# Second MoE of a fused attention and MoE kernel: the first unit's layer one is placed ahead of the other expert's folding, and fewer constant products stand among the first MoE's weight pieces

## The chip, the cores and the metric

The kernel runs on one core of a Trainium2 chip. It is one program: attention, a soft MoE over its output, and a top-1 MoE over that. The metric is the device time of one execution in microseconds (us), median of several runs; lower is better. TensorE (PE) does the matrix products, VectorE (DVE) and ScalarE (ACT) the elementwise work and the copies out of PSUM, GpSimd (POOL) some elementwise work and the indirect DMAs, SyncE (SP) issues the weight loads.

## The reference

```python
def _moe_ref(x, phi, w1, w2):            # first MoE, 8 experts, 4 slots each
    logits = x @ phi                     # x is the attention output, 3072 x 512
    d = softmax of logits over the tokens
    slot_input = (d.T @ x).reshape(E, S_per_e, D)
    for e in range(E):
        slot_out[e] = np.maximum(slot_input[e] @ w1[e], 0.0) @ w2[e]
    c = softmax of logits over the slots
    return c @ slot_out.reshape(n_slots, D)

def _moe2_ref(x, w_gate, w1, w2):        # second MoE, 8 experts, top 1
    logits = x @ w_gate
    expert_idx = np.argmax(logits, axis=1)
    gate_w = softmax(logits)[token, expert_idx]
    for e in range(E):
        mask = expert_idx == e           # experts without tokens are skipped
        out[mask] = gate_w[mask, None] * (np.maximum(x[mask] @ w1[e], 0.0) @ w2[e])
    return out
```
(shortened: the softmaxes are written in words.) w1 is 512 x 1024 and w2 is 1024 x 512 for each expert; each is 2 MB.

## The kernel before

**The first MoE's end.** Its weights come as 16 pieces of 2 MB (pieces 0 to 15), in order, through a ring of ten slots. Pieces 0 to 3 and 8 to 11 are first-layer weights (products at line 910), 4 to 7 and 12 to 15 second-layer weights (line 938). SP issues a load once its slot is free; a piece's products wait for its slot in `here(i)`. Ahead of that wait, for the pieces from 10 on, `here` issues 14 products of two constant tiles (`busy(14)`, line 836), whose result nobody reads. A product of f32 tiles shows in the trace as two records, so 14 of them read as x28 and 8 products of a piece as x16. After the last piece come ACT's copy of the result, four small products (line 954) and DVE's copy into `STR`, the 32 slot outputs.

**The second MoE's input is never formed.** A token's input is c (32 weights) times the slot outputs, so an expert's first layer is folded: G = slot outputs @ w1 of the expert, 32 rows (held as high and low parts in 128 partitions), and a token tile's hidden values are c @ G. Routing (DVE, lines 1607 to 1685) finds the experts in use, sorts the tokens by expert and makes units of 256 tokens, two tiles each. With this input two experts are in use, and there are 13 units. The weight loads (`v1`, first layer; `v2`, second layer) start when the experts are known, in the order v1 of expert 0, v1 of expert 1, v2 of expert 0, v2 of expert 1.

What PE does in order, with the lines of the kernel before:

1. `sort` (line 1411), 24 products with 42 columns: the tokens' numbers in sorted order. POOL then gathers the unit's rows of c from DRAM (line 1364, two indirect DMAs of 128 rows a unit).
2. Folding of both experts: per expert 8 products (line 1461), ACT copies the two halves out (line 1511), 2 products add the parts (line 1467), ACT writes the high part (line 1514), DVE the low part (line 1708).
3. `turn(0)` (line 1419), which transposes the gathered rows; the sort's second half with the gates (line 1411, 84 columns); `hidden(0)` (line 1427), the first unit's layer one. It waits for ACT's copy of the turned rows (line 1520) and of G into `Gst` (`fetch`, line 1540).
4. For each unit: tile 0 of the second layer, 24 products (lines 1490 to 1492) in four groups of six; inside it `turn(u + 1)`; after it `hidden(u + 1)`; then tile 1, 24 products. A group of tile 0 waits for its quarter of the hidden values (ACT's relu, line 1528, then DVE's low part, line 1714) and, with a new expert, for its quarter of the weights in high and low part (`high_in_place` on ACT, line 1551; `rest_in_place` on DVE, line 1721).

ACT and DVE have their orders written out by hand as well. On ACT, after the folding: `turned_out(0)`, `fetch(0)`, then the high parts of expert 0's second layer between the four relus, `fetch(e1)`, the four high parts of expert 1, and only then the loop over units, which begins with `turned_out(1)`. On DVE: routing, gates (lines 1688 to 1698), low parts of the folding, then low parts of hidden values and weights in turn, the final gates (1731, 1732), four low parts of expert 1's weights, and the loop over units.

Of the kernel before, what the change touches and what calls it, by code (L numbers as in the profile page):

```python
# [15 lines left out]
F32 = mybir.dt.float32  # L16
# [7 lines left out]
P = 128  # L24
# [646 lines left out]
def soft_moe(nc, ctx, sb, psum, sem, block, attended, mem, xmem, X, ident, ones, Rsel, phi_sb, load_piece,  # L671
# [134 lines left out]
    def _(pe):  # L806
# [327 lines left out]
def top1_moe(nc, ctx, sb, psum, sem, block, sp_passed, ident, ones, Rsel, wg_sb, mem, STR, CT, counting,  # L1134
# [27 lines left out]
    hh, hl = [work[:, i * HC:(i + 1) * HC].rearrange("p (q t) -> p q t", q=4) for i in range(2)]  # L1162
# [41 lines left out]
    sf = sb(st, "sf", [P, 3, MAXT])  # L1204

# [3 lines left out]
    def first_weights(odd):  # L1209

        return w2h[:, 1, :].bitcast(F32) if odd else raw
# [29 lines left out]
    v1_loaded = [sem("v1_loaded_even"), sem("v1_loaded_odd")]  # L1241
# [16 lines left out]
    g_here = sem("g_here")  # L1258
    act_passed = sem("act_passed")
# [20 lines left out]
    def count(eng):  # L1280

        return eng.value_load(rt[0:1, 5, 0:1], min_val=1, max_val=NE)
# [23 lines left out]
    def pairs_of(used):  # L1306


        return (used + 1) >> 1

    def load_v1(sp, e, odd):

        sp.dma_start(first_weights(odd).rearrange("p (c f) -> p c f", c=DC),
                     v1_d[bass.ds(e, 1)].rearrange("a (c p) f -> p (a c) f", p=P)).then_inc(v1_loaded[odd], 16)

    @block.sync
    def _(sp):
        sp.wait_ge(experts_known, 1)
        for odd in range(2):
            load_v1(sp, entry(sp, odd, 0), odd)  # L1320
        for r in range(2):
            load_v2(sp, entry(sp, r, 0), w2l[:, r, :].bitcast(F32), v2_loaded[r])
        used = count(sp)
        with sp.If(used > 2):
            with sp.Fori(1, pairs_of(used)) as i:
                for odd in range(2):
                    e = entry(sp, i * 2 + odd, 0)

                    sp.wait_ge(gp_done, i * 4 + 2 * odd)
                    sp.sem_inc(sp_passed, 1)  # L1330
                    load_v1(sp, e, odd)
            with sp.Fori(2, used) as r:
                e = entry(sp, r, 0)

                sp.wait_ge(w2_low, r * W2CH)
                sp.sem_inc(sp_passed, 1)
                load_v2(sp, e, raw, v2_loaded[1])

    @block.gpsimd
    def _(pool):  # L1340
        pool.sem_inc(y_quarter, 4)
        pool.sem_inc(y_scaled, 2)
        pool.sem_inc(gp_done, 2)
        pool.sem_inc(g_low, 2)
# [56 lines left out]
    def _(pe):  # L1401
# [20 lines left out]
        def hidden(u):  # L1422

            pe.wait_ge(cgt_out, u + 1)
            pe.wait_ge(g_here, u + 1)
# [25 lines left out]


        used = count(pe)
        with pe.Fori(0, pairs_of(used)) as i:
            pe.wait_ge(g_low, i * 4 + 2)
            for odd in range(2):
                pe.wait_ge(v1_loaded[odd], (i + 1) * 16)
                for half in range(2):
                    for c in range(DC):
                        at = c * F + half * 512  # L1460
                        mm = pe.matmul(Gp[c * SLOTS:(c + 1) * SLOTS, 2 * odd + half, :], STR[:, c, 0, :],
                                       first_weights(odd)[:, at:at + 512], start=True, stop=True,
                                       tile_position=(0, c * SLOTS))
                    mm.then_inc(gp_done, 1)
                for half in range(2):
                    pe.wait_ge(gp_out, i * 4 + 2 * odd + half + 1)
                    pe.matmul(Gp[:, 2 * odd + half, :], Rsel[:].rearrange("p r s -> p (r s)"),
                              Gpart[:, 2 * odd + half, :], start=True, stop=True).then_inc(g_done, 1)
        turn(0)
        pe.wait_ge(gates_hot, 1)  # L1470
        sort(slice(1, 3), slice(MAXT, 3 * MAXT))
        pe.wait_ge(g_low, pairs_of(used) * 4 + 2)
        hidden(0)
        pe.wait_ge(rt_ready, 1)
        with pe.Fori(0, used) as rank:
            units, first = entry(pe, rank, 1), entry(pe, rank, 2)
            high, low = [w[:, bass.ds(rank & 1, 1), :].rearrange("p a f -> p (a f)") for w in (w2h, w2l)]
            with pe.Fori(0, units) as j:

                u = first + j  # L1480
                for i in range(2):
                    pe.wait_ge(y_scaled, u * 2 + (i + 1))
                    for fc in range(FC):
                        if i == 0 and fc % 2 == 0:
                            pe.wait_ge(hid_low, u * 4 + (fc // 2 + 1))
                            pe.wait_ge(w2_low, rank * W2CH + (fc * D // CW + 1))
                        cols = slice(fc * D, (fc + 1) * D)
                        tokens = slice(fc % 2 * 2 * P + i * P, fc % 2 * 2 * P + (i + 1) * P)
                        h, rest = hh[:, fc // 2, tokens], hl[:, fc // 2, tokens]
                        pe.matmul(Yq[i][:], h, high[:, cols], start=(fc == 0), stop=False)  # L1490
                        pe.matmul(Yq[i][:], h, low[:, cols], start=False, stop=False)  # L1491
                        mm = pe.matmul(Yq[i][:], rest, high[:, cols], start=False, stop=(fc == FC - 1))  # L1492
                        if i == 0 and fc == 1:
                            turn(u + 1)
                        if i == 1 and fc % 2:
                            mm.then_inc(y_quarter, 1)
                    if i == 0:
                        mm.then_inc(y_first, 1)
                        hidden(u + 1)

    @block.scalar
    def _(act):
# [4 lines left out]
        with act.Fori(0, pairs_of(used)) as i:  # L1507
            for odd in range(2):
                for half in range(2):
                    act.wait_ge(gp_done, i * 4 + 2 * odd + half + 3)  # L1510
                    nc.scalar.copy(Gpart[:, 2 * odd + half, :], Gp[:, 2 * odd + half, :]).then_inc(gp_out, 1)
                for half in range(2):
                    act.wait_ge(g_done, i * 4 + 2 * odd + half + 1)
                    nc.scalar.copy(Gall[:, bass.ds(rank_at(i * 2 + odd), 1), half * 512:(half + 1) * 512].rearrange(
                        "p a f -> p (a f)").bitcast(F32R), Gp[:, 2 * odd + half, :]).then_inc(g_high, 1)
# [27 lines left out]
        act.wait_ge(rt_ready, 1)  # L1543
        e1 = act.value_load(tr[0:1, 1:2], min_val=0, max_val=NE - 1)
        act.wait_ge(g_low, pairs_of(used) * 4 + 2)
        act.sem_inc(act_passed, 1)

# [5 lines left out]

        turned_out(0)
        fetch(0)
        high_in_place(0, 0)
        for q in range(4):
            relu(0, q)
            if q < 3:
                high_in_place(0, q + 1)  # L1560
        fetch(e1)
        for ch in range(W2CH):
            high_in_place(1, ch)
# [21 lines left out]
    def _(dve):  # L1585
# [100 lines left out]

        dve.wait_ge(r_exp, 1)
# [12 lines left out]
        used = count(dve)  # L1700
        with dve.Fori(0, pairs_of(used)) as i:
            for odd in range(2):
                for half in range(2):
                    dve.wait_ge(g_high, i * 4 + 2 * odd + half + 1)
                    dve.sem_inc(dve_passed, 1)
                    rest = Gall[HD:P, bass.ds(rank_at(i * 2 + odd), 1), half * 512:(half + 1) * 512].rearrange(
                        "p a f -> p (a f)")
                    v.tensor_tensor(rest.bitcast(F32R), Gp[HD:P, 2 * odd + half, :], rest, ALU.subtract
                                    ).then_inc(g_low, 1)

        def low(u, q):

            dve.wait_ge(hid_high, u * 4 + (q + 1))
            v.scalar_tensor_tensor(hl[:, q, :], Gp[:, q, :], 0.0, hh[:, q, :].bitcast(F32),  # L1714
                                   ALU.max, ALU.subtract).then_inc(hid_low, 1)

        def rest_in_place(r, ch):

            dve.wait_ge(w2_high, r * W2CH + ch + 1)
            w = w2l[:, r, chunk(ch)]  # L1720
            v.tensor_tensor(w, w.bitcast(F32), w2h[:, r, chunk(ch)].bitcast(F32), ALU.subtract).then_inc(w2_low, 1)  # L1721

        for q in range(4):
            if q == 0:
                low(0, 0)
            rest_in_place(0, q)
            if q < 3:
                low(0, q + 1)
# [83 lines left out]
```

## Time and profile before

| | us |
|---|---|
| median of 3 runs | 462.95 (462.3 to 464.25) |
| profiled execution | 462.75 |
| its span in the trace | 461.0 |
| PE busy | 441.8 (96%) |
| DVE busy | 240.2 (52%) |
| ACT busy | 213.7 (46%) |
| POOL busy | 203.4 (44%) |

The page's line of the granted TensorE clock reads, over 40 equal slices of 11.5 us, `9999999999999999999999897799999999999999` in tenths of full speed. The span begins with the first instruction and ends with the last; the device time holds 1.75 us more around it. A busy PE may be waiting in the sense that matters: products of constant tiles count as busy. In a row of the trace the columns are start, length, engine, line, operation, result and operands, and in brackets the idle time ahead of it and what ended it. Records of PE overlap, since its ends are modelled; the chain of waits counts each stretch once.

### The profile page before, as it was taken

To read this page: it belongs to the slowest core of one execution; us is meant where nothing else is said; L and a number is where in the kernel's file an instruction comes from. 1 tells how busy PE (TensorE), PEld (TensorE's weight loads), DVE (VectorE), ACT (ScalarE), POOL (GpSimd) and SP (SyncE) were. 2 spreads that over 40 slices of the span, in tenths; PEclk is the share of its full clock that TensorE was granted. 3 is DMA by queue.
4 is the path that set the end of the run, shared out by engine and by line. 5 is a ranking of instruction groups with operands and counts; after the bars stand their busy time and mean duration, and the time that the engine had idled before them with its cause. 6 is when DMAs were issued, how large, how long until landed. Compare 5 with 4: busy or idle time off the path is not lost.

```text
span 461.0 us, 9685 instructions
## 1 busy us (share of the span) xinstructions
PE 441.8 (96%) x3152; PEld 370.7 (80%) x3153; DVE 240.2 (52%) x789; ACT 213.7 (46%) x419; POOL 203.4 (44%) x170
## 2 busy tenths in 40 slices
PE   8799999999999997999999989799999999999994
PEld 8689999999999995543567883688888888888883
DVE  6467677777677764665000386764333333333344
ACT  2578878788878763311010003853333232332243
POOL 3999888888888600020001001234333333333322
PEclk9999999999999999999999897799999999999999
DMA  8699898977676206999995059411111111111211
GB/s 233 261 411 370 338 386 305 381 267 253 213 254 217 66 2 204 383 401 408 390 384 162 1 202 383 169 36 57 57 57 57 57 57 45 46 57 54 54 49 13
DMA packets 27222, 89.21 MB, mean 194 GB/s; under 512 B 3280, under 2 KB 3280, under 8 KB 27184
## 3 DMA queue, kind: packets, MB, share of 16 engines
q1 hardware_dynamic: 23664, 78.47, 45.6%
q0 software_dynamic: 3360, 9.83, 6.9%
q10 hardware_dynamic: 160, 0.42, 0.4%
q8 instruction: 22, 0.36, 0.3%
q14 instruction: 16, 0.13, 0.1%
HBM read 80.85 MB, written 8.13 MB: 193 GB/s over the span
## 4 chain that ended last, share of the span: by engine, by line
PE 86%; DVE 5%; POOL 4%; ACT 1%; issue 1%; DMA 1%; SPq 0%; ACTq 0%; DVEq 0%; POOLq 0%
PE O L404 15%; PE Yq L1490 11%; PE Yq L1492 10%; PE Yq L1491 10%; PE PT L386 7%; PE Lp L836 4%; PE S L377 4%; PE S L376 4%; PE Lp L938 3%; PE Gp L1427 3%; PE XTp L819 2%; POOL kl L336 2%; PE Up L910 2%; POOL qs L332 2%; PE Up L828 1%
## 5 line engine op out<-in xcount | busy, mean ns | idle before, releaser
L461 ACT ACTIVATE shared<-shared,nm 128x256 f32<-128x256 f32 (+1 forms) x192 | 84.1, 486 | 32.6 <-DVE nm L564 32.6
L404 PE MATMUL O<-V,PTs 128*128 128x65 f32 x704 | 90.1, 269 | 1.1 <-ACT PTs L487 1.1
L404 PEld LDWEIGHTS O<-V,PTs 128*128 128x128 f32 x704 | 86.5, 191 | 2.4 <-ACT PTs L487 1.7
L564 DVE CUSTOM_DVE_ANT_0 shared<-S,TA 128x256 f32<-128x256 f32 (+1 forms) x192 | 68.8, 396 | 37.2 <-PE S L377 34.6
L1490 PE MATMUL Yq<-w2h,work 128*128 x208 | 83.3, 400 | 2.2 <-DVE w2l L1721 2.2
L1492 PE MATMUL Yq<-w2h,work 128*128 x208 | 82.1, 395 | 0.0
L1491 PE MATMUL Yq<-w2l,work 128*128 x208 | 82.1, 395 | 0.0
L1714 DVE SCALAR_TENSOR_TENSOR work<-Gp,work 128x512 fp32r<-128x512 f32 x56 | 38.6, 690 | 43.9 <-ACT work L1528 41.8
L336 POOL TENSOR_TENSOR kl<-k_raw,kh 128x1632 fp32r<-128x1632 f32 x15 | 55.2, 3679 | 9.3 <-ACT kh L471 9.1
L376 PE MATMUL S<-kh,qs 128*128 128x256 f32 (+1 forms) x180 | 53.0, 317 | 2.1 <-POOL kl L336 2.1
L386 PE MATMUL PT<-ident,shared 128*128 128x128 f32 x352 | 54.7, 274 | 0.0
L332 POOL TENSOR_TENSOR qs<-q_raw,qs 64x1536 fp32r<-64x1536 f32 x15 | 52.1, 3471 | 1.2
L1528 ACT ACTIVATE work<-Gp 128x512 fp32r<-128x512 f32 x56 | 33.6, 601 | 31.3 <-PE Yq L1492 29.6
L1750 DVE TENSOR_SCALAR mem<-Yq,gate_s 128x512 f32<-128x512 f32 x26 | 19.5, 751 | 54.8 <-PE Yq L1492 48.4
L1490 PEld LDWEIGHTS Yq<-w2h,work 128*128 128x128 f32 x208 | 39.6, 190 | 9.9 <-issue 2.4
L1492 PEld LDWEIGHTS Yq<-w2h,work 128*128 128x128 f32 x208 | 39.6, 190 | 8.5
L377 PE MATMUL S<-kl,qs 128*128 128x256 f32 (+1 forms) x180 | 46.2, 280 | 0.0
L1491 PEld LDWEIGHTS Yq<-w2l,work 128*128 128x128 f32 x208 | 39.7, 191 | 7.6
L1540 ACT CAST Gst<-mem 128x512 fp32r (+1 forms) x30 | 17.2, 621 | 58.8 <-PE Gp L1427 58.8
L1389 POOL DMA_INDIRECT out<-mem,dst x25 | 25.3, 1014 | 39.4 <-DVE mem L1750 29.5
L386 PEld LDWEIGHTS PT<-ident,shared 128*128 128x128 f32 x352 | 42.2, 156 | 0.4 <-ACT shared L461 0.3
L376 PEld LDWEIGHTS S<-kh,qs 128*128 128x128 f32 x180 | 34.1, 189 | 2.6 <-issue 2.6
(237 smaller groups left out, 593.3 us busy)
## 6 DMA issues: line engine op xcount, KB each, us to landing
mem<-in_moe_w SPq DMA_DIRECT2D x9, 2048.0 KB, 10.9
ext<-in_moe_w SPq DMA_DIRECT2D x6, 2048.0 KB, 19.3
k_raw<-in_k SPq DMA_DIRECT2D x15, 816.0 KB, 7.1
q_raw<-in_q SPq DMA_DIRECT2D x15, 768.0 KB, 5.5
V<-in_v SPq DMA_DIRECT2D x16, 715.0 KB, 5.7
xmem<-in_moe_w SPq DMA_DIRECT2D x2, 2048.0 KB, 12.3
w2l<-in_moe_w SPq DMA_DIRECT2D x2, 2048.0 KB, 20.8
w2h<-in_moe_w SPq DMA_DIRECT2D x1, 2048.0 KB
```

The lines of the kernel that those rows point to most:

```text
L332: nc.gpsimd.tensor_tensor(qs[HD:P, buf], q_raw[HD:P, buf], qs[HD:P, buf].bitcast(F32), ALU.subtract).then_inc(q_split, 1)
L336: nc.gpsimd.tensor_tensor(kl[:, buf], k_raw[:, buf], kh[:, buf].bitcast(F32), ALU.subtract).then_inc(k_split, 1)
L376: pe.matmul(S[par][h][:, 0:w], q, kh[:, buf, h, at:at + w], start=True, stop=False)
L377: mm = pe.matmul(S[par][h][:, 0:w], q, kl[:, buf, h, at:at + w], start=False, stop=True)
L386: mm = pe.transpose(PT[par][:, (h * kbs + kb) * P:(h * kbs + kb + 1) * P], Pb[:, par, h, kb * P:(kb + 1) * P], ident[:])
L404: mm = pe.matmul(O[grp % 2][:, at:at + VC], PTs[:, par, (h * kbs + kb) * P:(h * kbs + kb + 1) * P], V[:, buf, h, vb, :], start=(n == 0), s ...
L461: nc.scalar.activation(Pb[:, par, h, 0:width(g)], Pb[:, par, h, 0:width(g)], ACT.Exp, bias=nm[:, par, h:h + 1], scale=-1.0).then_inc(exp_d ...
L564: v.tensor_tensor_reduce(Pb[:, par, h, 0:w], S[par][h][:, 0:w], tab, -SCALE, HUGE, ALU.add, ALU.min, nm[:, par, h:h + 1]).then_inc(biased, 1)
L1490: pe.matmul(Yq[i][:], h, high[:, cols], start=(fc == 0), stop=False)
L1491: pe.matmul(Yq[i][:], h, low[:, cols], start=False, stop=False)
L1492: mm = pe.matmul(Yq[i][:], rest, high[:, cols], start=False, stop=(fc == FC - 1))
L1714: v.scalar_tensor_tensor(hl[:, q, :], Gp[:, q, :], 0.0, hh[:, q, :].bitcast(F32), ALU.max, ALU.subtract).then_inc(hid_low, 1)
```

## The change

Four things change.

- **Constant products among the weight pieces.** `here` issues 8 of them ahead of pieces 14 and 15 only, in place of 14 ahead of each of pieces 10 to 15. In the sort, two constant products stand between the groups of four.
- **The order of folding on PE.** Expert 0 is folded alone, its G goes straight to `Gst` (which `hidden(0)` reads), and its layer one and tile 0 of unit 0 come next. Expert 1's folding, the sort with the gates, `turn(1)` and `hidden(1)` stand between tile 0 and tile 1 of unit 0. Two groups of four constant products stand around `turn(0)` and `hidden(0)`. ACT keeps expert 0's G in `Gall` by one copy of 1024 columns. The folding's products and their sums use different PSUM halves.
- **The orders of ACT and DVE** follow: expert 0's first high part comes ahead of `turned_out(0)`, the second right behind it; the gates on DVE move behind the first unit's low parts.
- **The loads** are issued in the order v1, v2 of expert 0, v1, v2 of expert 1. The hidden values `hh` and `hl` have memory of their own instead of sharing it with the sort's tiles.

The core of the diff:

```diff
         def here(i):
-            if i >= NSLOT:
-                busy(14, STp)
+            if i >= len(PIECES) - 2:
+                busy(8, STp)
             pe.wait_ge(slot_loaded[i % NSLOT], 16 * (i // NSLOT + 1))
...
-        for odd in range(2):
-            load_v1(sp, entry(sp, odd, 0), odd)
         for r in range(2):
-            load_v2(sp, entry(sp, r, 0), w2l[:, r, :].bitcast(F32), v2_loaded[r])
+            e = entry(sp, r, 0)
+            load_v1(sp, e, r)
+            load_v2(sp, e, w2l[:, r, :].bitcast(F32), v2_loaded[r])
...
             for t in range(TT):
                 if t % REP == 0:
+                    if which.start == 0 and t:
+                        busy(2)
                     pe.wait_ge(hot_done, t // REP + 1)
...
+        fold(0)
+        busy(4)
+        turn(0)
+        hidden(0)
+        busy(4)
+        pe.wait_ge(rt_ready, 1)
         used = count(pe)
...
+        first = halves_of(entry(pe, 0, 2))
+        tile(0, 0, 0, *first)
+        with pe.If(used > 1):
+            with pe.Fori(1, used) as r:
+                fold(r)
         pe.wait_ge(gates_hot, 1)
         sort(slice(1, 3), slice(MAXT, 3 * MAXT))
...
+        turn(1)
+        pe.wait_ge(g_low, used * 2)
+        hidden(1)
+        tile(0, 1, 0, *first)
...
# ScalarE
+        high_in_place(0, 0)
+        turned_out(0)
+        high_in_place(0, 1)
+        for q in range(4):
+            relu(0, q)
+            if q < 2:
+                high_in_place(0, q + 2)
+        nc.scalar.copy(Gall[:, 0, :], Gst[:].bitcast(F32)).then_inc(g_kept, 1)
+        with act.If(used > 1):
+            with act.Fori(1, used) as r:
+                fold(r)
         act.wait_ge(rt_ready, 1)
         e1 = act.value_load(tr[0:1, 1:2], min_val=0, max_val=NE - 1)
-        act.wait_ge(g_low, pairs_of(used) * 4 + 2)
+        act.wait_ge(g_low, used * 2)
         act.sem_inc(act_passed, 1)
...
+        act.wait_ge(g_kept, 1)
         fetch(e1)
+        act.wait_ge(v1_loaded[1], 16)
         for ch in range(W2CH):
             high_in_place(1, ch)
...
# VectorE
+        fold(0)
+        rest_in_place(0, 0)
+        for q in range(4):
+            low(0, q)
+            if q < 3:
+                rest_in_place(0, q + 1)
         dve.wait_ge(r_exp, 1)
         step(v.tensor_reduce(gate[:], E2[:], AX, ALU.add))
...
+        with dve.If(used > 1):
+            with dve.Fori(1, used) as r:
+                fold(r)
```

Three places of the orders follow. First PE at the last weight pieces; a row is line, operation, result, operands, shape and count, `-` before and `+` after the change, and L836 is the constant product, L910 and L938 the products of the pieces.

```order
-L910 MATMUL Up<-mem,LT 32x512 x8
-L836 MATMUL Lp<-ones,ident 128x128 x14
-L910 MATMUL Up<-mem,LT 32x512 x8
+L910 MATMUL Up<-mem,LT 32x512 x16
 L922 MATMUL XTp<-ident,xmem 128x128 x8
-L836 MATMUL Lp<-ones,ident 128x128 x14
-L938 MATMUL Lp<-mem,xmem 32x512 x8
-L836 MATMUL Lp<-ones,ident 128x128 x14
-L938 MATMUL Lp<-mem,xmem 32x512 x8
-L836 MATMUL Lp<-ones,ident 128x128 x14
+L938 MATMUL Lp<-mem,xmem 32x512 x16
+L836 MATMUL Lp<-ones,ident 128x128 x8
```

The constant products ahead of pieces 10 to 13 are gone, and those ahead of 14 are 8 instead of 14.

Next PE behind the sort. Before the change (L1461 and L1467 fold, here expert 1's part and its end; L1419 is `turn(0)`, L1411 the sort with the gates):

```order
L1461 MATMUL Gp<-w2h,shared 32x512 [waits v1_loaded_odd]
L1461 MATMUL Gp<-w2h,shared 32x512 x7
L1466 REGISTER_ALU
L1467 MATMUL Gp<-mem,Rsel 128x512 [waits gp_out]
L1466 REGISTER_ALU
L1467 MATMUL Gp<-mem,Rsel 128x512 [waits gp_out]
L1454 ISA
L1454 COMPARE_AND_BRANCH
L1419 MATMUL Cp<-ident,Cg 128x128 [waits gathered]
L1419 MATMUL Cp<-ident,Cg 128x128
L1411 MATMUL Sp<-work 128x84 [waits hot_done,gates_hot]
L1411 MATMUL Sp<-work 128x84 x3
```

And after it (L1460 and L1469 are expert 0's folding, L1398 constant products, L1414 `turn(0)`, L1425 `hidden(0)`):

```order
L1460 MATMUL Gp<-mem,shared 32x512 [waits v1_loaded_first]
L1460 MATMUL Gp<-mem,shared 32x512 x7
L1469 MATMUL Gp<-mem,Rsel 128x512 [waits gp_out] x2
L1398 MATMUL Cp<-ones,ident 128x128 x4
L1414 MATMUL Cp<-ident,Cg 128x128 [waits gathered]
L1414 MATMUL Cp<-ident,Cg 128x128
L1425 MATMUL Gp<-CgT,Gst 128x256 [waits g_low,cgt_out]
L1425 MATMUL Gp<-CgT,Gst 128x256 x7
L1398 MATMUL Cp<-ones,ident 128x128 x4
```

The turn now stands one expert's folding earlier, and layer one right behind it; the other folding and the sort with the gates have moved behind tile 0.

Last ACT after the change, from three of expert 1's high parts (L1586) to the copy of unit 1's turned rows (L1560, `turned_out(1)`), which PE's `hidden(1)` waits for; what lies between reads registers for the loops.

```order
L1586 CAST w2h<-w2l 128x1024 [waits v2_loaded_second] x3
L1609 UNCONDITIONAL_BRANCH
L1609 ISA
L1278 TENSOR_LOAD rt
L1278 ISA x3
L1278 TENSOR_LOAD rt
L1278 ISA x2
L1611 UNCONDITIONAL_BRANCH
L1611 ISA
L1572 TENSOR_LOAD tr
L1572 ISA x2
L1560 CAST CgT<-Cp 128x256 [waits cg_turned]
```

Within ACT this piece reads as before. What moved is what is ahead of it: expert 1's folding now comes directly ahead of the fetch and the four high parts, where before it came ahead of unit 0's layer one.

## Rows read from the trace of the kernel before

**Rows 1.** Chain of waits at the last pieces: start, length, what ran.
```profile
251.27 3.32 PE Lp L836 x28
254.59 1.85 PE Lp L938 x16
256.44 0.87 PE XTp L951 x6
```

**Rows 2.** Timeline of SP: issues of pieces 14 and 15.
```profile
214.75 10.45 SPq L109 DMA_DIRECT2D ext<-in_moe_w  x1
225.24 5.29 SPq L109 DMA_DIRECT2D ext<-in_moe_w  x1
```

**Rows 3.** DMA issues alone in their window: size, us to landing (pieces 14, 15).
```profile
ext<-in_moe_w SPq DMA_DIRECT2D x1, 2048.0 KB, 24.7
ext<-in_moe_w SPq DMA_DIRECT2D x1, 2048.0 KB, 19.4
```

**Rows 4.** Windows by engine: us, busy (x) of PE, PEld, DVE, ACT, POOL; PEclk, DMA share, GB/s.
```profile
276.10:282.90 6.80, 6.80 (x29) 3.35 (x29) 5.74 (x22) 1.17 (x2) 1.98 (x2) 0.50 1.01 384
293.20:299.90 6.70, 4.99 (x13) 3.92 (x14) 6.70 (x9) 6.70 (x10) 1.46 (x2) 0.50 0.04 12
303.20:461.00 157.80, 151.86 (x729) 126.65 (x727) 58.45 (x82) 52.66 (x92) 56.00 (x86) 1.00 0.16 50
```

**Rows 5.** Chain of waits from the sort to the second tile of unit 0.
```profile
274.07 4.40 PE Sp L1411 x24
278.47 3.57 PE Gp L1461 x16
...
284.40 1.85 PE Gp L1461 x16
286.25 1.93 PE Gp L1467 x4
...
289.13 0.70 DVE mem L1708
...
290.23 1.15 ACT Gst L1540 x2
...
296.55 0.43 PE Yq L1490
...
303.22 0.94 PE Gp L1427 x8
304.16 0.23 PE Yq L1490
```

**Rows 6.** Timeline of POOL: unit 0's second gather DMA, and the wait for unit 1's gather.
```profile
281.02 0.94 POOL L1364 DMA_INDIRECT Cg<-c_rows,src_i  x1 [0.30 <-issue]
...
295.84 0.60 POOL L1358 COPY src<-src_i 128x2 int32 x1 [4.47 <-DMA Cg<-c_rows,src_i]
```

**Rows 7.** Timeline of DVE, PE and ACT from the sort to unit 0.
```profile
273.33 3.69 DVE L1666 TENSOR_TENSOR work<-ab,col 128x512 fp32r<-128x512 f32 x6
288.14 2.85 PE L1411 MATMUL Sp<-work 128*128 128x84 f32 x24
291.27 1.05 ACT L1551 CAST w2h<-w2l 128x1024 fp32r<-128x1024 f32 x1
292.21 0.60 ACT L1528 ACTIVATE work<-Gp 128x512 fp32r<-128x512 f32 x1
292.84 0.69 DVE L1714 SCALAR_TENSOR_TENSOR work<-Gp,work 128x512 fp32r<-128x512 f32 x1 [3.02 <-ACT work L1528]
294.58 0.69 DVE L1714 SCALAR_TENSOR_TENSOR work<-Gp,work 128x512 fp32r<-128x512 f32 x1
294.91 0.79 PE L1490 MATMUL Yq<-w2h,work 128*128 x1 [2.22 <-DVE w2l L1721]
298.01 3.92 ACT L1551 CAST w2h<-w2l 128x1024 fp32r<-128x1024 f32 x4
301.81 0.39 ACT L1520 CAST CgT<-Cp 128x256 fp32r<-128x256 f32 x1
```

More of the change, by code:

```diff
@@ L1424, in hidden @@
             pe.wait_ge(cgt_out, u + 1)
-            pe.wait_ge(g_here, u + 1)
+            if isinstance(u, int) and u == 0:
+                pe.wait_ge(g_low, 2)
+            else:
+                pe.wait_ge(g_here, u)
             for fc in range(FC):
@@ L1450, in _ @@
         sort(slice(0, 1), slice(0, MAXT))
-        used = count(pe)
[L1454 to L1468, printed above, removed]
@@ L1469, in _, with fold @@
-        turn(0)
+        def fold(r):
+            later = not isinstance(r, int)
+            if later:
+                pe.wait_ge(v1_loaded[1], r * 16)
+            else:
+                pe.wait_ge(v1_loaded[0], 16)
+            for half in range(2):
+                for c in range(DC):
+                    at = c * F + half * 512
+                    mm = pe.matmul(Gp[c * SLOTS:(c + 1) * SLOTS, half, :], STR[:, c, 0, :],
+                                   first_weights(later)[:, at:at + 512], start=True, stop=True,
+                                   tile_position=(0, c * SLOTS))
+                mm.then_inc(gp_done, 1)
+            if later:
+                pe.wait_ge(g_low, r * 2)
+            for half in range(2):
+                pe.wait_ge(gp_out, r * 2 + (half + 1))
+                pe.matmul(Gp[:, 2 + half, :], Rsel[:].rearrange("p r s -> p (r s)"),
+                          Gpart[:, half, :], start=True, stop=True).then_inc(g_done, 1)
@@ new lines, in tile @@
+        def tile(u, i, rank, high, low):
+            pe.wait_ge(y_scaled, u * 2 + (i + 1))
+            for fc in range(FC):
+                if i == 0 and fc % 2 == 0:
+                    pe.wait_ge(hid_low, u * 4 + (fc // 2 + 1))
+                    pe.wait_ge(w2_low, rank * W2CH + (fc * D // CW + 1))
+                cols = slice(fc * D, (fc + 1) * D)
+                tokens = slice(fc % 2 * 2 * P + i * P, fc % 2 * 2 * P + (i + 1) * P)
+                h, rest = hh[:, fc // 2, tokens], hl[:, fc // 2, tokens]
+                pe.matmul(Yq[i][:], h, high[:, cols], start=(fc == 0), stop=False)
+                pe.matmul(Yq[i][:], h, low[:, cols], start=False, stop=False)
+                mm = pe.matmul(Yq[i][:], rest, high[:, cols], start=False, stop=(fc == FC - 1))
+                if i == 0 and fc == 1 and not isinstance(u, int):
+                    turn(u + 1)
+                if i == 1 and fc % 2:
+                    mm.then_inc(y_quarter, 1)
+            if i == 0:
+                mm.then_inc(y_first, 1)
@@ new lines, in halves_of, with unit_products @@
+        def halves_of(rank):
+            return [w[:, bass.ds(rank & 1, 1), :].rearrange("p a f -> p (a f)") for w in (w2h, w2l)]
+        def unit_products(u, rank, high, low):
+            tile(u, 0, rank, high, low)
+            hidden(u + 1)
+            tile(u, 1, rank, high, low)
+        fold(0)
[4 more added lines that the diff above has]
+        pe.wait_ge(rt_ready, 1)
+        used = count(pe)
+        first = halves_of(entry(pe, 0, 2))
+        tile(0, 0, 0, *first)
@@ L1470, in _ @@
+        with pe.If(used > 1):
+            with pe.Fori(1, used) as r:
+                fold(r)
         pe.wait_ge(gates_hot, 1)
         sort(slice(1, 3), slice(MAXT, 3 * MAXT))
[L1472 to L1499, printed above, removed]
@@ new lines, in _ @@
+        turn(1)
+        pe.wait_ge(g_low, used * 2)
+        hidden(1)
+        tile(0, 1, 0, *first)
+        units = entry(pe, 0, 1)
+        with pe.If(units > 1):
+            with pe.Fori(1, units) as j:
+                unit_products(j, 0, *first)
+        with pe.If(used > 1):
+            with pe.Fori(1, used) as rank:
+                units, first = entry(pe, rank, 1), entry(pe, rank, 2)
+                with pe.Fori(0, units) as j:
+                    unit_products(first + j, rank, *halves_of(rank))
@@ L1506, in _, with fold @@
         used = count(act)
[L1507 to L1515, printed above, removed]
+        def fold(r):
+            for half in range(2):
+                act.wait_ge(gp_done, r * 2 + (half + 1))
+                nc.scalar.copy(Gpart[:, half, :], Gp[:, half, :]).then_inc(gp_out, 1)
+            for half in range(2):
+                cols = slice(half * 512, (half + 1) * 512)
+                act.wait_ge(g_done, r * 2 + (half + 1))
+                if isinstance(r, int):
+                    g = Gst[:, cols]
+                else:
+                    act.sem_inc(act_passed, 1)
+                    g = Gall[:, bass.ds(rank_at(r), 1), cols].rearrange("p a f -> p (a f)").bitcast(F32R)
+                nc.scalar.copy(g, Gp[:, 2 + half, :]).then_inc(g_high, 1)
+        fold(0)
         def turned_out(u):
@@ L1698, in _ @@
         v.tensor_tensor(dst_i[:], src_i[:], sf[:, 0, :], ALU.add).then_inc(dst_ready, 1)
[L1700 to L1728, printed above, removed]
+        with dve.If(used > 1):
+            with dve.Fori(1, used) as r:
+                fold(r)
         dve.wait_ge(sorted_done, 2)
```

60 lines of the change are left out of this document (36 added, 24 removed).

## The prediction

> **What bounds the kernel now.** I read the row of busy shares first (PE 96%), then the chain of waits, then windows for the granted clock. From 303.2 us on, the clock is 1.00 and PE is busy for 151.86 of 157.80 us [rows 4]; those are the products of units 0 to 12, which the change leaves alone. So whatever the change does shows in when tile 1 of unit 0 starts, 304.16 us before [rows 5], and all later times move with it. Ahead of that point the chain is PE's own through the last weight pieces, but it runs through constant products: 14 of them took 3.32 us, the piece's own products 1.85 [rows 1]. Behind the sort the chain changes engine often, and the clock stands at 0.50 twice, from 276.1 to 282.9 and from 293.2 to 299.9 [rows 4].
>
> I count in the times of the trace before, and part the change at the end of the last piece and at the end of the sort.
>
> **Term A, the constant products.** The loads set a floor. Piece 14 was issued at 214.75 and landed 24.7 us later, at 239.45; piece 15 at 225.24 + 19.4 = 244.64 [rows 2, 3]. Their slots were free long before, by pieces 4 and 5, which the change doesn't touch, so these landings stay. Piece 13 should land one such pitch (5.2) ahead of 14, at 234.3. Before, PE took up piece 15 at 254.59 [rows 1], 9.95 us after it had landed: constant products had pushed it there, no wait. Without those of pieces 10 to 13, four pieces cost 4 x 1.85 = 7.4 us, plus the turning of the hidden values between 11 and 12; PE then waits for 13, and ends it at 234.3 + 1.85 = 236.1. Eight constant products (8/14 x 3.32 = 1.90) end at 238.0, ahead of 14's landing; piece 14 ends at 241.3, the next eight at 243.2, ahead of 15's. Piece 15 starts some 0.15 behind its landing, at 244.8, and ends at 246.65 instead of 256.44: **-9.8**. What is late next is the load itself; not all 6 x 3.32 = 19.9 us of constant products are won. The other end of the range: PE now idles some 1.5 us ahead of each of the last pieces, and if that takes its clock to half, piece 15 costs 1.85 more, A is -7.9. It can't be more than -9.95. I take -9.8, since PE still works two thirds of that time.
>
> **Term B, the sort.** Before, DVE wrote the six groups by 273.33 + 3.69 = 277.02, and PE ended at 278.47, at half clock from 276.1 on [rows 4, 5, 7]. The change puts 5 x 2 constant products between: at 3.32/14 = 0.237 each 2.4 us at full clock, twice that at half. At full clock throughout the six groups (4 products of about 0.12, as in the constant products' records) and these need 274.07 + 6 x 0.48 + 2.4 = 279.3, that is +0.8. PE idles ahead of the sort as before, so I expect the clock still to fall in it; with about half of the rest at half clock the sort ends at 281.0, **+2.5**. If it stays at half to the end, 282.6, +4.1. Call the sort's end E.
>
> **Term C, from E to the first tile.** Expert 0's folding takes 1.85 + 1.93 = 3.8 us of PE at full clock [rows 5] (5.9 before, at half), four constant products 0.95, so PE is ready for `turn(0)` at E + 4.8. It now waits for the gather. Before, that was hidden: expert 1's folding lay over it, and the gather's landing can only be bounded: its second DMA ended on POOL at 281.96 (E + 3.5) [rows 6], and the turn could begin behind the folding, at 288.2 (E + 9.7) [rows 5]. By the early end PE would not wait at all and the turn would come at E + 4.8, 3.2 us sooner than I take; by the late one, 1.7 later. The nearest row is the next unit's gather, awaited for 4.47 us behind its issue, while weights were loading too [rows 6]. I take that one: E + 3.5 + 4.47 = E + 8.0. Then turn and ACT's copy, `hidden(0)` at E + 9.0. ACT has a high part (1.05) between the copy and the first relu, so relu (0.60) ends at about E + 10.6, DVE's low part (0.69) at E + 11.3, and tile 0 starts at **E + 11.4**. Before it was 294.91 - 278.47 = 16.4 [rows 5, 7]. So this part gains 5 us. G needs no fetch (1.15) [rows 5], and no weight is waited for: v2 of expert 0 is second in the queue instead of third.
>
> The Trainium skill ("DMA: Bandwidth & Descriptors", the section with a DMA's two cost components) puts a fixed cost of about 2.0 us on a DMA and the rest on its bytes. By that, an estimate, the gather of 64 KB lands near E + 5.6 and the sum is 2.4 us less, as in rival 1. The row shows 4.47 us, with weights loading beside it.
>
> **Term D, tile 0.** DVE has a low part of the hidden values and one of the weights per group; their pitch was 294.58 - 292.84 = 1.74 us [rows 7]. A group of six products takes 6 x 0.23 = 1.4 us at full clock, so DVE sets the pace: X = E + 11.4 + 3 x 1.74 + 1.4 = **E + 18.0**. Before, 303.22 - 278.47 = 24.75. At half clock a product took 0.43 [rows 5], a group takes 2.6, and PE sets the pace, X = E + 21.6. Constant products run on either side of `hidden(0)`, so the clock may be back by then; I take full.
>
> **Term E, from X to tile 1; here the change loses.** Before, `hidden(1)` followed at once and tile 1 started 0.94 later [rows 5]. Now expert 1's folding begins at X. From the start of a folding at full clock (284.40) to the end of the last low part (289.83) it is 5.4 us [rows 5]. ACT then fetches G (1.15), and its next four instructions are expert 1's high parts (3.92), and only behind them the copy of unit 1's turned rows (0.39) [rows 5, 7]. PE wants that copy for `hidden(1)`. PE has 3.8 us of folding, 2.85 of sort [rows 7] and the turn, and is through at X + 7; the copy ends at X + 10.9. So PE waits 4 us, `hidden(1)` starts at X + 11.0 and tile 1 at **X + 11.9**. The sort and both foldings were paid before as well, but in C's 16.4 us. The cover of the four high parts was tile 0, 8.3 us of PE; that cover is gone. DVE has its gates done by then, and the final gates and four low parts end near X + 12.5, ahead of the next unit's need.
>
> The clock will stand at half behind such a wait. Before, PE was idle for 2.22 us ahead of 294.91 [rows 7], and the clock stayed at 0.50 until 299.9 [rows 4], 5.0 us into the tile, which cost 2.5 us. It could also be back at full before the copy comes, a cost of 0. The new wait is the longer one, but a clock that has fallen early is back early; I take 1.7, nearer to the row.
>
> **Sum.** Tile 1 starts at E + 18.0 + 11.9 = E + 29.9, before E + 25.7, so +4.2; clock +1.7; B +2.5; A -9.8. Together -1.4. From the span 461.0 that gives 459.6, with 1.75 outside it **461.4 us** for an execution like the profiled one (462.75, 0.2 below the median 462.95 of the runs). A measurement tells 0.5% (2.3 us) from no change, so this counts as no change.
>
> **Rivals.**
> 1. *The first unit comes early, and the loss is small.* The gather lands before PE asks for it (C -3.2), the constant products hold the clock in the sort (B +0.8 in place of +2.5, -1.7) and behind the wait for the copy (-1.7). For it: the constant products stand where the clock fell. Against: 4.47 us in rows 6, and the idle time ahead of the sort is unchanged. All would give 454.8, half of it **458.1**.
> 2. *Slower: PE stays at half clock through unit 0.* Waiting for the gather, then for the copy, PE runs tile 0 at 2.6 us a group. Price +3.6 in D, and the second wait costs clock as in the 2.5 above, +0.8; **465.8**. It decides once more than two groups of tile 0 run at half. For it: behind the wait of 2.22 us tile 0 took 303.22 - 294.91 = 8.3 us before, where 24 x 0.23 = 5.5 would do. Against: DVE's pace hides 0.35 us of each group's loss, and constant products fill part of the wait.
> 3. *The reordering costs nothing,* because the copy's wait isn't there as I read it or something shortens it; only A is left: 461.0 - 9.8 + 1.75 = **453**. ACT's order speaks against it.
> 4. *The constant products aren't won,* because PE's clock falls at the last pieces and stays down through the small products: A -7.9, **463.3**, still no change.
>
> **Numbers.** Forecast 0.36 (own range 459.5 to 463.5), rival 1 0.28, rival 2 0.22, rival 3 0.05, rival 4 0.09. Rival 1 and 3 and a small part of the forecast fall below 460.6: faster 0.35. Rival 2 above 465.3, with a little of the rest: slower 0.23. The rest, 0.42, is no change. Adding all the unkind ends (+4.4, +1.9, B +1.6, C +1.7) gives 471, all the kind ones 455; the range that leaves out 2 in 10 is 457.0 to 466.5.
>
> **What would show it.** A: the last L938 products end near 246.7 with a wait of PE on a DMA ahead. B: sort's end less its start 5 to 8.5 us. C: PE idle ahead of L1414, 2 to 4 us, put down to the gather; tile 0 within 12 us of the sort's end. E: PE idle some 4 us ahead of `hidden(1)`, released by ACT's copy L1560, which follows four L1586; the clock at 0.50 behind it. The prediction is wrong if PE doesn't wait there, if the gather lands by E + 6, or if units 1 to 12 take another time than before from tile 1's start to the end, 461.0 - 304.16 = 156.8 us plus what the clock takes.

## Result: 0.7% slower, where no change was forecast

| | us |
|---|---|
| before, median of 6 runs | 463.52 (462.3 to 464.37) |
| after, median of 6 runs | 466.2 (465.38 to 468.21) |
| ratio after to before | 1.0068 (95% interval 1.0041 to 1.0096) |
| profiled execution before, its span | 462.75, 461.0 |
| profiled execution after, its span | 466.38, 464.6 |

The forecast was 461.4, and 466.2 lies inside its range (457.0 to 466.5), but the kernel became slower, clear of the interval, where slightly faster was forecast. The span grew by 3.6 us where -1.4 was forecast.

The timeline of PE in the changed kernel; the columns are start, length, engine, line, operation, operands, count, and in brackets the idle time ahead and what ended it. L938 are a piece's products, L1406 the sort, L1460 the folding, L1414 a turn, L1425 a layer one, L1482 the first of each three products of the second layer.

```profile
244.41 1.92 PE L938 MATMUL Lp<-ext,xmem 128*32 128x512 f32 x16 [1.38 <-DMA ext<-in_moe_w]
...
263.96 0.62 PE L1406 MATMUL Sp<-work 128*128 128x42 f32 x4 [1.47 <-DVE work L1711]
...
271.98 3.64 PE L1460 MATMUL Gp<-mem,shared 128*32 128x512 f32 x16
...
280.06 0.44 PE L1414 MATMUL Cp<-ident,Cg 128*128 128x128 f32 x2 [1.50 <-DMA Cg<-c_rows,src_i]
280.96 1.21 PE L1425 MATMUL Gp<-CgT,Gst 128*128 128x256 f32 x8 [0.46 <-ACT CgT L1560]
...
283.38 0.49 PE L1482 MATMUL Yq<-w2h,hh 128*128 x1 [0.33 <-issue]
...
290.00 1.92 PE L1460 MATMUL Gp<-w2h,shared 128*32 128x512 f32 x16
...
301.09 2.05 PE L1425 MATMUL Gp<-CgT,Gst 128*128 128x256 f32 x8 [4.38 <-ACT CgT L1560]
...
310.19 0.39 PE L1482 MATMUL Yq<-w2h,hh 128*128 x1
...
316.00 1.11 PE L1425 MATMUL Gp<-CgT,Gst 128*128 128x256 f32 x8
...
328.37 1.11 PE L1425 MATMUL Gp<-CgT,Gst 128*128 128x256 f32 x8
```

The last piece waits for its load and ends at 246.33 in the chain of waits, instead of 256.44 [rows 1]. The sort takes until 271.98. Tile 0 runs from 283.38 to 290.00. Then PE waits 4.38 us for ACT's copy, as forecast. Unit 1 begins at 310.19. From one layer one to the next, 316.00 to 328.37, a unit takes 12.37 us.

What ACT did ahead of that copy, in its timeline: the fetch, expert 1's four high parts, the copy.

```profile
295.80 1.14 ACT L1580 CAST Gst<-mem 128x512 fp32r x2 [1.17 <-DVE mem L1744]
296.85 3.88 ACT L1586 CAST w2h<-w2l 128x1024 fp32r<-128x1024 f32 x4
300.63 0.36 ACT L1560 CAST CgT<-Cp 128x256 fp32r<-128x256 f32 x1
```

And POOL's last issue of unit 0's gather, which `turn(0)` waits for:

```profile
274.61 0.94 POOL L1357 DMA_INDIRECT Cg<-c_rows,src_i  x1 [0.30 <-issue]
```

Windows of the changed kernel, in the columns of [rows 4], which they answer to:

```profile
265.70:275.80 10.10, 10.10 (x48) 7.08 (x48) 3.38 (x15) 0.69 (x2) 1.98 (x2) 0.50 1.02 382
299.90:306.30 6.40, 5.21 (x16) 4.52 (x17) 3.47 (x4) 2.73 (x5) 0.34 (x2) 0.50 0.05 14
311.40:464.60 153.20, 147.48 (x692) 120.34 (x690) 53.61 (x76) 49.09 (x86) 54.62 (x83) 1.00 0.16 50
```

The clock was at half for 10 us, through all but the first 1.7 us of the sort and 3.8 us into the folding, and again behind the wait for the copy. From 311.4 on it is full, and PE as busy as before. Yet that stretch is longer. In PE's timeline of the kernel before two layers one lie 12.12 us apart:

```profile
315.14 1.11 PE L1427 MATMUL Gp<-CgT,Gst 128*128 128x256 f32 x8
...
327.26 1.11 PE L1427 MATMUL Gp<-CgT,Gst 128*128 128x256 f32 x8
```

To part the 3.6 us I take the chain of waits of both kernels, as the prediction did; it puts a start of PE up to 0.2 us later than the timeline. Its rows in the changed kernel, and last the start of unit 1 in the kernel before:

```profile
246.33 0.86 PE XTp L951 x6
...
271.38 0.69 PE Sp L1406 x4
...
303.14 0.43 PE Yq L1482
...
310.36 0.23 PE Yq L1482
```

```profile
309.63 0.23 PE Yq L1490
```

| stretch | before | after | difference |
|---|---|---|---|
| to the end of the last piece | 256.4 | 246.3 | -10.1 |
| from there to the sort's end, of it the sort 4.4 and 8.1 | 22.0 | 25.7 | +3.7 |
| sort's end to tile 1 of unit 0 | 25.7 | 31.1 | +5.4 |
| tile 1 of unit 0 | 5.5 | 7.2 | +1.8 |
| unit 1 to the end | 151.4 | 154.2 | +2.9 |

(Differences are worked out from unrounded rows.) The last line was nowhere in the forecast. The prediction had named it as a sign of being wrong: tile 1's start to the end took 161.5 us, 4.6 more than before, and the clock explains only some 1.6 of them.

### The profile page after: what moved, and what is told of

Its sections match the earlier page's. It is cut to its first block, busy times and chain, and to the rows that moved or that the text cites. A ratio compares the mean times of both kernels' runs of the same rounds, so it can differ in the third digit from the quotient of the medians.

```text
span 464.6 us, 9268 instructions
## 1 busy us (share of the span) xinstructions
PE 437.4 (94%) x3052; PEld 362.2 (78%) x3053; DVE 240.0 (52%) x789; ACT 213.2 (46%) x418; POOL 202.2 (44%) x170
## 4 chain that ended last, share of the span: by engine, by line
PE 80%; DMA 7%; POOL 5%; DVE 4%; issue 2%; ACT 2%; ACTq 0%; SPq 0%; DVEq 0%; POOLq 0%
PE O L404 15%; PE Yq L1482 11%; PE Yq L1483 11%; PE Yq L1484 11%; PE PT L386 7%; PE S L377 4%; DMA ext<-in_moe_w 4%; PE S L376 4%; PE Gp L1425 3%; PE XTp L819 3%; PE Cp L1398 2%; PE Lp L938 2%; POOL kl L336 2%; POOL qs L332 1%; PE Up L828 1%
## 5 line engine op out<-in xcount | busy, mean ns | idle before, releaser
L1482 PE MATMUL Yq<-w2h,hh 128*128 x208 | 84.3, 405 | 0.5 <-issue 0.3
L1483 PE MATMUL Yq<-w2l,hh 128*128 x208 | 82.9, 399 | 0.0
L1484 PE MATMUL Yq<-w2h,hl 128*128 x208 | 82.8, 398 | 0.0
L1749 DVE SCALAR_TENSOR_TENSOR hl<-Gp,hh 128x512 fp32r<-128x512 f32 x56 | 38.5, 688 | 47.0 <-ACT hh L1568 47.0
L1568 ACT ACTIVATE hh<-Gp 128x512 fp32r<-128x512 f32 x56 | 33.5, 601 | 34.7 <-PE Yq L1484 34.6
L1482 PEld LDWEIGHTS Yq<-w2h,hh 128*128 128x128 f32 x208 | 39.6, 190 | 10.3 <-issue 1.9
L1484 PEld LDWEIGHTS Yq<-w2h,hl 128*128 128x128 f32 x208 | 39.4, 190 | 9.7
L1483 PEld LDWEIGHTS Yq<-w2l,hh 128*128 128x128 f32 x208 | 39.5, 190 | 8.3
L1580 ACT CAST Gst<-mem 128x512 fp32r x28 | 16.0, 618 | 61.2 <-PE Gp L1425 60.0
```

## Experiments

Two questions: do the terms of the forecast hold when each part stands alone, and what makes each unit 0.25 us longer, which over the 12 units from unit 1 on is the 2.9 us? The theory for the second was the memory of `hh` and `hl`: by the allocation they began 32 bytes off a multiple of 64 before (within `work`), like the weights `w2h` and `w2l`, and begin at a multiple of 64 now. The rivals were the part of the memory, and the new loop's code.

**e1, the constant products among the pieces alone.**

```diff
# on the kernel before
-            if i >= NSLOT:
-                busy(14, STp)
+            if i >= len(PIECES) - 2:
+                busy(8, STp)
```

> The kernel before with one edit: 8 constant products ahead of pieces 14 and 15, none ahead of 10 to 13. Theory (constant products had pushed the last pieces behind their landing; the second MoE does not care): the last piece's products end at 246.4 instead of 256.4 and everything behind keeps its distances, so 462.9 - 10.1 = about 453, ratio 0.978. Rival (the loads or a clock at half take it back): the last piece ends later, or the distance from there to the end grows by several us: 457 or more.

Measured: 452.63, ratio 0.9762 (0.9711 to 0.9813). Its chain of waits at the last piece:

```profile
225.97 19.41 DMA ext<-in_moe_w
245.42 1.92 PE Lp L938 x16
247.35 0.87 PE XTp L951 x6
```

The chain now steps from the last load to its products; the constant products are off it. The theory holds, and this one edit is worth some 11 us: it beats both kernels. In this trace 9.1 us of it stand at the last piece (247.35 against 256.44); the rest comes behind it, where the clock stood at half for less time than in the kernel before (3.4 and 6.9 us against 6.8 and 6.8).

**e2, hh and hl in memory of their own, in the kernel before.**

```diff
# on the kernel before
-    hh, hl = [work[:, i * HC:(i + 1) * HC].rearrange("p (q t) -> p q t", q=4) for i in range(2)]
...
     sf = sb(st, "sf", [P, 3, MAXT])
+    hh, hl = [sb(st, n, [P, 4, HC // 4], F32R) for n in ("hh", "hl")]
```

> The kernel before with one edit: hh and hl have memory of their own behind sf, where the changed kernel has them, instead of lying in work. Theory (their place makes each product of the second layer 6 ns longer, which is why a unit takes 12.37 us in the changed kernel and 12.12 before): a unit takes 12.37 us, the whole about 3.2 us longer, 466, ratio 1.007. Rival (something else in the changed loop, its code or its waits, makes the unit longer): a unit takes 12.12 us and the time stays at 463.

Measured: 467.18, ratio 1.0072 (1.0041 to 1.0103). Two layers one in PE's timeline:

```profile
316.95 1.11 PE L1427 MATMUL Gp<-CgT,Gst 128*128 128x256 f32 x8
...
329.33 1.11 PE L1427 MATMUL Gp<-CgT,Gst 128*128 128x256 f32 x8
```

12.38 us a unit, in the loop's code of the kernel before. So it is the memory, not the loop.

**e3, 32 bytes ahead of hh in the changed kernel.**

```diff
# on the changed kernel
+    sb(st, "pad", [P, 8])
     hh, hl = [sb(st, n, [P, 4, HC // 4], F32R) for n in ("hh", "hl")]
```

> The changed kernel with 32 bytes a partition left free ahead of hh, so that hh and hl begin 32 bytes off a multiple of 64, as in the kernel before; they still lie in the last part of the memory. Theory alignment: a unit takes 12.12 us again, 463. Theory place (the part of the memory): a unit takes 12.37, 466.2. Theory that memory has nothing to do with it: 12.37 too, and then the kernel before with own memory must show 12.12.

Measured: 463.71, ratio 0.9997 (0.9972 to 1.0023). Timeline of PE:

```profile
315.94 1.11 PE L1426 MATMUL Gp<-CgT,Gst 128*128 128x256 f32 x8
...
328.06 1.11 PE L1426 MATMUL Gp<-CgT,Gst 128*128 128x256 f32 x8
```

12.12 us again, with nothing moved but `hh` and `hl`, by 32 bytes.

**e5 and e6, the same 32 bytes in the kernel before,** ahead of `work`, and ahead of `w2h`, which lies two tensors earlier.

```diff
# e5, on the kernel before
+    sb(st, "pad", [P, 8])
     work = sb(st, "work", [P, TT * (P + 3 * MAXT)], F32R)
# e6, on the kernel before
+    sb(st, "pad", [P, 8])
     w2h = sb(st, "w2h", [P, 2, WSIZE], F32R)
```

> The kernel before with 32 bytes a partition left free ahead of work, in which hh and hl lie: they now begin at a multiple of 64 bytes, and the second-layer weights w2h and w2l still 32 bytes off one. Theory (start of the stationary tile against a multiple of 64, wherever it lies in the memory): a unit takes 12.37 us instead of 12.12 and the time is 466. Rival (it is the last part of the memory that is slow at some places, and e3 moved hh out of such a place): a unit stays at 12.12, 463.

> The kernel before with the same 32 bytes ahead of w2h, so that w2h, w2l, hh and hl all begin at a multiple of 64 bytes. Theory relative (stationary and moving tile must start alike): a unit takes 12.12 us, 463. Theory absolute, of the stationary tile: 12.37 as in e5, 466. If the moving tile's own start counts too, another value than both.

Measured: e5 467.08, ratio 1.0062 (1.0031 to 1.0093); e6 464.66, ratio 1.0015 (0.9986 to 1.0043). PE's timeline of e5:

```profile
317.18 1.12 PE L1428 MATMUL Gp<-CgT,Gst 128*128 128x256 f32 x8
...
329.54 1.11 PE L1428 MATMUL Gp<-CgT,Gst 128*128 128x256 f32 x8
```

and of e6:

```profile
315.01 1.11 PE L1428 MATMUL Gp<-CgT,Gst 128*128 128x256 f32 x8
...
327.14 1.11 PE L1428 MATMUL Gp<-CgT,Gst 128*128 128x256 f32 x8
```

12.36 and 12.13 us. In e5 `hh` lies low in the memory and is slow, so the part of the memory doesn't explain it. In e6 all four tiles begin at a multiple of 64 and the unit is fast, so that multiple isn't slow by itself. What goes with the slow unit is that the stationary tile (`hh`, `hl`) and the streamed one (`w2h`, `w2l`) start differently modulo 64 bytes:

| kernel | `hh`, `hl` | `w2h`, `w2l` | unit, us |
|---|---|---|---|
| before, e3 | 32 | 32 | 12.12 |
| changed, e2 | 0 | 32 | 12.37, 12.38 |
| e5 | 0 | 32 | 12.36 |
| e6 | 0 | 0 | 12.13 |

(The starts modulo 64 are worked out from the order and sizes of the tensors in the kernels, not read from a trace.) The paddings of e5 and e6 move everything behind them, but it is the second layer's products that differ: from 335 to 435 us they come every 0.235 us in the changed kernel, e2 and e5, and every 0.230 us in the kernel before, e3 and e6, while a layer one takes 0.94 to 0.95 us in all. The relative theory held in all of these. In every slow case the two are off by just 32 bytes; that 64 is the unit, and not a larger power of two, is not shown, nor is it which of the four tiles counts. Why it costs time stays open too.

**e4, the copy of the turned rows ahead of the four high parts.**

```diff
# ScalarE, on the changed kernel
         fetch(e1)
+        turned_out(1)
         act.wait_ge(v1_loaded[1], 16)
...
-                turned_out(u + 1)
+                with act.If(u > 0):
+                    turned_out(u + 1)
```

> The changed kernel with ACT's copy of unit 1's turned rows ahead of expert 1's four high parts (and skipped in the loop's first pass). Theory (the copy's place in ACT's order is what PE waits 4.4 us for): hidden(1) starts 3.6 us earlier, some 7.4 us behind the end of tile 0, and the clock falls for less: 466.2 - 3.6 to - 5.5, so 460.7 to 462.6. Rival (what is late next, the four high parts and DVE's low parts ahead of the first low part of unit 1, takes it back): hidden(1) is earlier, but unit 1's tile 0 starts less than 2 us earlier, 465.

Measured: 465.64, ratio 1.0045 (1.0017 to 1.0073), against 1.0068 for the changed kernel. PE's timeline, from `hidden(1)` on:

```profile
297.93 1.19 PE L1425 MATMUL Gp<-CgT,Gst 128*128 128x256 f32 x8 [0.62 <-ACT CgT L1560]
...
306.26 0.51 PE L1482 MATMUL Yq<-w2h,hh 128*128 x1 [1.55 <-DVE hl L1751]
...
313.68 0.50 PE L1482 MATMUL Yq<-w2h,hh 128*128 x1 [2.74 <-DVE hl L1751]
```

and DVE's, ahead of those waits:

```profile
298.89 4.63 DVE L1758 TENSOR_TENSOR w2l<-w2l,w2h 128x1024 fp32r<-128x1024 f32 x4 [1.37 <-ACT w2h L1586]
304.86 0.75 DVE L1803 TENSOR_SCALAR mem<-Yq,gate_s 128x512 f32<-128x512 f32 x1 [1.34 <-issue]
...
312.28 0.75 DVE L1803 TENSOR_SCALAR mem<-Yq,gate_s 128x512 f32<-128x512 f32 x1 [4.88 <-DMA out<-mem,dst]
312.95 0.68 DVE L1751 SCALAR_TENSOR_TENSOR hl<-Gp,hh 128x512 fp32r<-128x512 f32 x1
```

The wait for the copy fell from 4.38 us to 0.62, and two others took its place, 1.55 and 2.74. DVE runs expert 1's four low parts first and scales tile 0's output behind them; tile 1's scaling then waits 4.88 us for the store of tile 0, since both use one buffer, and unit 1's last low part stands behind it. The theory is confirmed for the wait: `hidden(1)` comes 7.3 us behind the end of tile 0 (290.60) instead of 11.1, and the clock reads 1.00 from 297.9 to 312.0, so it no longer falls there. It fails for the gain, and the rival, which had the high and DVE's low parts take it back, is right in kind. It named the wrong place, though: unit 1's tile 0 starts 3.9 us earlier (306.26 against 310.19), and the time goes in the last group of that tile. From the end of tile 0 to unit 2's layer one (315.19) 1.4 us are left. The medians' ratios differ by 1 us and their intervals overlap, so that the whole is faster is not shown.

**e7, the changed kernel with e3's padding and without the constant products in the sort.**

```diff
# on the changed kernel, beside the padding of e3
                 if t % REP == 0:
-                    if which.start == 0 and t:
-                        busy(2)
                     pe.wait_ge(hot_done, t // REP + 1)
```

> The changed kernel with the padding of e3 and without the two constant products between the groups of the sort. Theory (all of them were at half clock and on PE's path: the sort took 8.0 us instead of 4.4): the sort takes 4.4 us, 3.6 less, folding at half clock as it is now, so 463.7 - 3.6 = 460.1. Rival (they gave part of that back by keeping the clock up later): the sort is shorter, but more of the folding and of layer one runs at half, 461.5 or more.

Measured: 460.16, ratio 0.9915 (0.9885 to 0.9946). PE's timeline:

```profile
265.74 4.81 PE L1405 MATMUL Sp<-work 128*128 128x42 f32 x24 [1.47 <-DVE work L1710]
270.48 3.43 PE L1459 MATMUL Gp<-mem,shared 128*32 128x512 f32 x16
...
300.59 2.05 PE L1424 MATMUL Gp<-CgT,Gst 128*128 128x256 f32 x8 [4.38 <-ACT CgT L1559]
```

and that of e3, which has them:

```profile
263.94 0.62 PE L1407 MATMUL Sp<-work 128*128 128x42 f32 x4 [1.47 <-DVE work L1712]
...
272.93 2.81 PE L1461 MATMUL Gp<-mem,shared 128*32 128x512 f32 x16
...
302.22 2.04 PE L1426 MATMUL Gp<-CgT,Gst 128*128 128x256 f32 x8 [4.41 <-ACT CgT L1561]
```

The time is the theory's (460.1). The sort takes 4.7 us instead of 9.0, and from its start to `hidden(1)` it is 34.9 us instead of 38.3. The sort's constant products cost 3.8 us by the ratios (0.9997 - 0.9915, of 463; the intervals don't touch) and 3.4 us in the traces. What is left of the change against e1, that is the new orders with the order of the loads and the eight constant products around `turn(0)` and `hidden(0)`, costs 0.9915 - 0.9762, about 7 us.

**e8, the sort's constant products in e1.**

```diff
# on e1
                 if t % REP == 0:
+                    if which.start == 0 and t:
+                        busy(2)
                     pe.wait_ge(hot_done, t // REP + 1)
```

> The kernel of e1 (before, with fewer constant products among the pieces) with two constant products between the groups of the sort, as the changed kernel has. Theory: the sort takes some 8 us instead of 3.75, the folding of both experts comes later by that, and the time is 452.6 + 3.6 to 4.3 = 456.5. Rival (the clock gets back to full sooner and the folding and layer one gain it back): 453 to 454.5.

Measured: 455.39, ratio 0.981 (0.9749 to 0.9872). PE's timeline of e8, then of e1:

```profile
263.98 0.62 PE L1413 MATMUL Sp<-work 128*128 128x42 f32 x4 [1.48 <-DVE work L1668]
...
272.78 3.02 PE L1463 MATMUL Gp<-mem,shared 128*32 128x512 f32 x16
...
295.85 1.11 PE L1429 MATMUL Gp<-CgT,Gst 128*128 128x256 f32 x8
```

```profile
264.26 3.75 PE L1411 MATMUL Sp<-work 128*128 128x42 f32 x24 [1.47 <-DVE work L1666]
268.26 3.28 PE L1461 MATMUL Gp<-mem,shared 128*32 128x512 f32 x16 [0.26 <-issue]
...
291.69 1.11 PE L1427 MATMUL Gp<-CgT,Gst 128*128 128x256 f32 x8
```

The folding starts 4.5 us later, layer one of unit 1 4.2 us later. From the sort's start to that layer one it is 31.9 us in e8, 27.4 in e1 and 28.3 in e10, which is e1 once more: 3.6 or 4.4 us by the traces. The medians differ by 2.8 us and their intervals overlap, so by them alone neither sign nor size is settled; the traces give the sign, and it agrees with e7.

What the constant products did to the clock shows in windows of e8 and of e1, in the columns of [rows 4]:

```profile
264.80:275.00 10.20, 10.20 (x52) 8.53 (x54) 4.84 (x18) 0.21 (x1) 0.94 (x1) 0.50 1.02 399
```

```profile
267.70:271.00 3.30, 3.04 (x18) 0.80 (x17) 2.96 (x14) 0.59 (x1) 1.48 (x2) 0.50 1.02 413
```

It is the same in all traced executions: with constant products in the sort (changed kernel, e3, e4, e8) the clock stands at half for 10.2 us from early in the sort on, and the sort takes 8.0 to 9.0 us; without them (the other eight) it stands there for 3.4 to 6.9 us, and the sort takes 4.0 to 4.7. Why is open.

**e9 and e10, no constant products at the pieces, and e1 again beside it.**

```diff
# e9, on the kernel before; e10 is e1
-            if i >= NSLOT:
-                busy(14, STp)
```

> The kernel before with no constant products at all among the weight pieces (e1 keeps 8 ahead of each of the last two). Theory (the landing of the last piece sets the end; the constant products only keep the clock): the last piece starts at its landing as in e1. If PE's clock falls in the longer idle times, its products and the small ones behind it run at half: 452.6 + 2 to 4. If not, 452.6 within noise.

> The kernel of e1 once more, beside e9 on the same chip and with more rounds: 452.6, ratio 0.976 to the kernel before. It is the fastest version so far, faster than both the kernel before and the changed one.

Measured: e9 453.34, ratio 0.9778 (0.9744 to 0.9812); e10 452.02, ratio 0.9755 (0.9723 to 0.9787). PE's timeline of e9:

```profile
245.37 3.23 PE L935 MATMUL Lp<-ext,xmem 128*32 128x512 f32 x16 [2.72 <-DMA ext<-in_moe_w]
248.53 0.94 PE L948 MATMUL XTp<-ones,ident 128*128 128x128 f32 x6
```

Without them the last piece took 3.23 us instead of 1.92, as its products ran partly at half clock, and it ended at 248.53; in e1 it was 247.28. On the whole the medians differ by 1.3 us and the intervals overlap, so what the 8 constant products buy on the whole is not shown. e10 repeats e1's gain; e1 and e9 are both clearly faster than the kernel before and the changed one.

## Why the prediction was wrong

**A, the constant products among the pieces: right.** -9.8 forecast, -10.1 in the trace, and e1 shows it alone. The clock read 1.00 from 230.0 to 246.3, so rival 4 did not happen.

**B, the sort: the mechanism right, the size off.** +2.5 was taken, between +0.8 and +4.1; it was +3.7. The clock fell at 265.7, 1.7 us into the sort, and did not return in it: the window from there to 275.8 reads 0.50. The ten constant products, meant to be at half clock in part, were so nearly all, and most of the folding (5.5 us instead of 3.8) too, which C had at full. e7 and e8 agree on the sign, e7 on the size. This execution was the mildest of the four with such a sort: e3's sort took 9.0 us, beyond the range's upper end.

**C and D, from the sort's end to tile 0's: right.** Turn at E + 8.1 (forecast 8.0), `hidden(0)` at E + 9.0 (9.0), tile 0 at E + 11.4 (11.4), its end at E + 18.0 (18.0). The gather's latency from the next unit's gather [rows 6] was the right choice: it was 4.5 us here, from the end of the last issue (275.55) to the turn. It also hid an error of C: PE was through with folding and constant products at E + 6.6, not E + 4.8, and waited only 1.50 us more. That every point fits to a tenth is luck of this execution: in e3 and e4 tile 0 ended at E + 18.2, in e7 at E + 19.0, since the gather there took 5.4 us. (At half clock D's sum gives E + 21.7, not 21.6.) By the price of the Trainium skill ("DMA: Bandwidth & Descriptors", the two cost components), a fixed part of about 2.0 us and the bytes, the gather would have landed near E + 5.7, an estimate; the 4.5 us of this trace don't agree with it.

**E, the wait for ACT's copy: right in place and length, the clock's part too small.** PE waited 4.38 us (4 forecast) and `hidden(1)` began at X + 11.1 (11.0). `hidden(1)` and tile 1 then took 9.1 us, to 310.19, instead of 6.4: 2.7 lost, nearly all to half clock, where 1.7 was taken. In e4, with the wait of 0.62 us, the clock stayed at full. What I had not seen is how little the wait is worth alone (e4): next in line stand DVE's low parts and the one buffer of the store.

**The failed step is the first one: "those are the products of units 0 to 12, which the change leaves alone".** The instructions are the same, but their operands moved: the section on the change names the new memory of `hh` and `hl`, and the prediction gave it no price. Twelve units of 48 products at 5 ns more are the 2.9 us that turned no change into a slower kernel. e2 shows it by the placement alone, e3, e5 and e6 with 32 bytes of padding. e3 is the direct check: the changed kernel with the old relation of the tiles has a ratio of 0.9997, the no change that was forecast, though 463.7 us and not 461.4. Together: B +1.2, the clock in E +1.0, placement +2.9, A -0.3, and 0.2 in small steps make the 5.0 us between -1.4 and +3.6.

Of the rivals, the slower one (PE at half clock through unit 0, 465.8) gave nearly the measured time for a reason that was mostly not its own: tile 0 ran at full clock (283.4 to 290.0), at DVE's pace. The first rival (the gather lands early, the constant products hold the clock) did not happen: in all four traces with them in the sort the clock stood at half for longer. The third (the reordering costs nothing) is refuted by e7 against e1, 7 us.

## What to carry to other kernels

A diff that gives a tile memory of its own can change every product that reads it, though no instruction changes: where the same products run hundreds of times, compare where the stationary and the streamed tile start before and after (here they came to lie 32 bytes apart modulo 64), and try a padding if that differs. Take each part of a bundle alone; here one edit of two lines was worth 11 us and the rest cost 14. Before constant products are put in to keep the clock up, look whether the next load or the next wait hides them: here eight ahead of each of the last two loads were hidden up to the landing, fourteen ahead of six pieces had pushed the end back by 10 us, and ten in the sort cost some 3 to 4 us, as they ran at half clock.

## What the runs showed of the hardware that was not expected

- Products of 128 x 128 by 512 columns (fp32r) whose stationary tile and streamed tile start 32 bytes apart modulo 64 make a unit 12.36 to 12.38 us long; with both at the same remainder, 0 or 32, it is 12.12 to 12.13. Per product, of 48 in a unit, that is 5 ns. No wait of PE shows from 312 us on in either kernel.
- The granted clock stayed at 0.50 for 10.1 us (265.7 to 275.8) while PE's records were busy for all 10.10 of them, with four records of products of 42 columns and four of constant products in turn, then with 3.8 us of the folding's products of 512 columns. In e8 it was the same for 10.20 us (264.8 to 275.0). In e1, whose sort has no constant products, the clock fell 3.4 us into the sort and stood at 0.50 for 3.4 us.
